# A new opening for a convolution and two fused MLPs on one core: taps by way of TensorE, the first convolution split between VectorE and TensorE

## The reference

```
w   = softmax(weight, axis=-1)                       # weight [8 heads, 7 taps]
out[b,s,h,g] = sum_k w[h,k] * x_pad[b, s+k, h, g]    # causal convolution over s, 24 channels a head
h1  = out.reshape(8192,192) @ w_in ;  g1 = max(0.01*h1, h1) ;  y1 = g1 @ w_out
h2  = y1 @ w_in2
g2  = h2 where h2>=1, 0 where h2<=-1, else (h2+1)**2/4
result = g2 @ w_out2                                 # d_model 192, d_ff 2048, x [2,4096,192] float32
```

## Time and profile before

| | |
|---|---|
| median of 3 runs | 1127.24 us (1127.17 to 1127.33) |
| the profiled execution | 1128.94 us, of which the span from first to last instruction is 1127.2 us |
| TensorE busy | 99% of the span, 9754 matmuls |
| VectorE busy | 80% |
| ScalarE busy | 71% |
| mean granted TensorE clock | 0.997 |

### The profile page before, as it was taken

The page is one execution under the profiler, slowest core; times in us unless marked ns, Lnnn a source line. Parts: engine busy times, 40 slices in busy tenths (PEclk is TensorE's granted clock), DMA queues, the critical chain, the costliest instruction groups (busy, mean ns, idle before and its releaser), DMA issues.

```text
span 1127.2 us, 25736 instructions
## 1 busy us (share of the span) xinstructions
PE 1117.2 (99%) x9754; PEld 923.7 (82%) x9754; DVE 898.4 (80%) x1511; ACT 798.7 (71%) x1472; POOL 45.8 (4%) x76
## 2 busy tenths in 40 slices
PE   8999999999999999999999999999999999999998
PEld 7888888888888888888888888888888888888886
DVE  6888887888777887788877888787788877888666
ACT  5878667586775867758577685866758677686785
POOL 4452000000000000000000000000000000000000
PEclk8999999999999999999999999999999999999999
DMA  6430010101001010010100101001010100100001
GB/s 132 109 77 6 14 17 1 30 2 25 6 1 30 1 29 1 1 30 1 29 1 8 23 1 29 1 13 18 1 29 1 24 7 1 29 1 15 1 1 29
DMA packets 114568, 21.98 MB, mean 19 GB/s; under 512 B 106256, under 2 KB 114448, under 8 KB 114448
## 3 DMA queue, kind: packets, MB, share of 16 engines
q1 hardware_dynamic: 111600, 19.61, 9.7%
q10 hardware_dynamic: 2848, 0.75, 0.4%
HBM read 14.05 MB, written 6.29 MB: 18 GB/s over the span
## 4 chain that ended last, share of the span: by engine, by line
PE 96%; DVE 2%; ACT 1%; issue 0%; DMA 0%; DVEq 0%
PE hidden L435 15%; PE hidden L429 10%; PE hidden L431 10%; PE hidden L433 10%; PE acc_main L499 10%; PE acc_main L501 10%; PE acc_edge L493 10%; PE acc_edge L490 10%; PE acc_main L503 10%; DVE g L958 0%; DVE acc_main L905 0%; ACT pre L681 0%; DMA y_main<-in_weight_dram 0%; ACT g_hi L700 0%; PE hidden L451 0%
## 5 line engine op out<-in xcount | busy, mean ns | idle before, releaser
L700 ACT CAST g_hi<-g 128x512 fp32r<-128x512 f32 x510 | 299.4, 618 | 267.6 <-PE acc_main L531 199.6
L969 DVE TENSOR_TENSOR g_lo<-g,g_hi 128x512 fp32r<-128x512 f32 x510 | 333.4, 687 | 94.3 <-ACT g_hi L700 89.7
L963 DVE SCALAR_TENSOR_TENSOR g<-hidden,pre 128x512 f32<-128x512 f32 x256 | 176.6, 690 | 101.6 <-ACT pre L688 98.7
L435 PE MATMUL hidden<-op_edge,w_edge 64*128 64x512 f32 x768 | 257.0, 388 | 0.0
L429 PE MATMUL hidden<-op_hi,w_main 64*128 64x512 f32 x512 | 198.6, 388 | 1.7 <-ACT op_hi L727 1.5
L447 PE MATMUL hidden<-op_hi,w_main 64*128 64x512 f32 x512 | 198.7, 388 | 0.0
L431 PE MATMUL hidden<-op_lo,w_main 64*128 64x512 f32 x512 | 198.7, 388 | 0.0
L451 PE MATMUL hidden<-op_hi,w_main 64*128 64x512 f32 x512 | 198.4, 388 | 0.0
L449 PE MATMUL hidden<-op_lo,w_main 64*128 64x512 f32 x512 | 198.4, 387 | 0.0
L433 PE MATMUL hidden<-op_hi,w_main 64*128 64x512 f32 x512 | 198.4, 387 | 0.0
L456 PE MATMUL hidden<-op_edge,w_edge 64*128 64x512 f32 x512 | 198.1, 387 | 0.0
(11 more groups left out here) (128 smaller groups left out, 2776.2 us busy)
## 6 DMA issues: line engine op xcount, KB each, us to landing
x_in<-in_x_dram SPq DMA_DIRECT2D x67, 64.0 KB, 2.2
out_dram<-y_main SPq DMA_DIRECT2D x62, 64.0 KB, 1.8
stage<-in_moe_w_out_dram SPq DMA_DIRECT2D x15, 192.0 KB, 2.7
x_in_edge<-in_x_dram SPq DMA_DIRECT2D x66, 32.0 KB, 2.0
out_dram<-y_edge SPq DMA_DIRECT2D x32, 64.0 KB, 1.8
stage<-in_moe_w_in_dram SPq DMA_DIRECT2D x15, 128.0 KB, 2.3
stage<-in_moe_w_in_dram SPq DMA_DIRECT2D x30, 64.0 KB, 2.4
stage<-in_moe_w_out_dram ACTq DMA_DIRECT2D x1, 192.0 KB, 4.2
```

The costliest lines, as they stand in the source:

```text
L435: done = nc.tensor.matmul(h[:], w_edge[l][top, i - 3, cols], op_edge[l][b][top, :], start=False, stop=False)
L700: nc.scalar.copy(hi_of(n, c)[:], g[c % SLOTS][:]).then_inc(g_hi_ready, 1)
L969: nc.vector.tensor_tensor(lo_of(n, c)[:], g[c % SLOTS][:], hi_of(n, c)[:].bitcast(F32), ALU.subtract).then_inc(g_lo_ready, 1)
```

## The change

The taps load brings 8x7 numbers to 8 partitions. GpSimd makes two 0/1 masks (`head_of`, 8 x 128); TensorE multiplies them with the raw taps, so that each of 128 partitions holds the logits of its own main and its own edge head. The softmax is then over 2x7 numbers a partition. The table of the exponential is called for by an early activation on a zero.

ScalarE scales `same` by the main taps (`main_diag`), and TensorE makes the last 128 columns of tile 0's main convolution; VectorE makes the first 384, and rounds these itself. GpSimd scales `same` by the edge taps. The warming matmuls are 3 ahead of the logits and 7 behind them. Piece 0 of the weights is loaded on SyncE's queue but for one part; half of tile 1's main x on ScalarE's. Chunk 0's edge passes (i = 3, 4) go ahead of its main passes. Of tile 1 one tap is made early and six in job 0; the parts of its operand are waited for pass by pass.

```
-WARM = 16
+WARM = 3
+WARM_ON = 7
+SPLIT = 3 * T // 4
-EARLY_TAPS = 2
-JOB_0_MAIN_TAPS = {0: 2, 1: 3, 2: 4, 3: 5, 4: 6}
-JOB_0_EDGE_TAPS = {6: (0,), 8: (1,), 9: (2, 3), 10: (4,), 11: (5, 6)}
+JOB_0_MAIN_TAPS = {0: 1, 1: 2, 2: 3, 3: 4, 4: 5, 5: 6}
+JOB_0_EDGE_TAPS = {8: (0, 1), 9: (2, 3), 10: (4,), 11: (5, 6)}
...
@@ sync
-                sp.dma_start(s[:, 0:PW], w[0:P]).then_inc(loaded, 16)
+                if piece:
+                    sp.dma_start(s[:, 0:PW], w[0:P]).then_inc(loaded, 16)
...
             load_x_edge(EVEN, 0, parts=range(2))
+            load_weights(0)
             load_weights(1)
-            load_x_main(ODD, 0)
+            load_x_main(ODD, 0, parts=P // Q - 2)
             load_weights(2)
@@ gpsimd
-            nc.gpsimd.memset(own[:], 1.0).then_inc(own_step, 1)
...
+            nc.gpsimd.memset(head_of, 1.0).then_inc(head_step, 1)
+            main = head_of[:, 0, :]
+            edge = head_of[:, 1, :].rearrange("h (r c) -> h r c", r=2)
+            pool.wait_ge(head_step, 1)
+            nc.gpsimd.affine_select(out=main, in_=main, compare_op=ALU.is_ge, fill=0.0, base=0,
+                                    pattern=[[1, P]], channel_multiplier=-GROUP)
...
+            pool.wait_ge(same_step, 3)
+            pool.wait_ge(taps_ready, 1)
+            for i in range(TAPS):
+                nc.gpsimd.tensor_scalar(edge_diag[i], same, taps[:, 1, i:i + 1], None, ALU.mult
+                                        ).then_inc(edge_diag_ready, 1)
+            low_w_in(0)
+            low_w_in(1)
+            low_w_out(0)
+            low_w_in(2)
+            low_w_out(1)
+            low_w_out(2)
@@ tensor: top_first
             if is_number(n, 0) and c == 0:
+                begin, last = i == 3, 1
+                if i == 3:
+                    pe.wait_ge(edge_hi_ready, 2)
+                    pe.wait_ge(weights_hi, 2)
+                if i == 4:
+                    pe.wait_ge(weights_ready, 1)
                 if i == 0:
                     pe.wait_ge(main_rounded, 1)
-                    pe.wait_ge(weights_hi, 1)
+                    pe.wait_ge(first_rounded, 1)
...
+            if is_number(n, 1) and c == 0:
+                if i == 0:
+                    pe.wait_ge(main_rounded, 2)
+                if i == 1:
+                    pe.wait_ge(main_low_ready, 1)
                 if i == 3:
-                    pe.wait_ge(edge_hi_ready, 2)
+                    pe.wait_ge(edge_hi_ready, 5)
@@ tensor: bottom_first, i == 3
-                if is_number(n, 0) and c == 0:
-                    pe.wait_ge(op1_ready, 1)
+                if is_number(n, 0, 1) and c == 0:
+                    pe.wait_ge(op1_ready, n + 1)
@@ tensor: opening
-            for i in (0, 2, 1, 3, 4):
+            for i in (3, 4, 0, 2, 1):
@@ tensor: ahead of the edge convolution
+            pe.wait_ge(head_of_ready, 1)
+            pe.wait_ge(taps_loaded, 16)
+            for a in (0, 1):
+                nc.tensor.matmul(logits[:, a, :], head_of[:, a, :], taps_raw, start=True, stop=True
+                                 ).then_inc(logits_ready, 1)
+            keep_warm(WARM_ON)
+            pe.wait_ge(x_turned, 1)
+            for i in range(TAPS):
+                pe.wait_ge(main_diag_ready, i + 1)
+                last = nc.tensor.matmul(last_main, main_diag[i], x_main[0][:, SPLIT + i:T + i],
+                                        start=i == 0, stop=i == TAPS - 1)
+            last.then_inc(last_convolved, 1)
@@ scalar
-            act.dma_start(taps_raw[:], weight.partition_broadcast(P)).then_inc(taps_loaded, 16)
+            act.dma_start(taps_raw, weight).then_inc(taps_loaded, 16)
...
+            act.wait_ge(warm_ready, 1)
+            nc.scalar.activation(exp_of_zero, g[0][:, 0:1], ACT.Exp)
...
             for i in range(TAPS):
-                nc.scalar.activation(edge_diag[i], same, ACT.Copy, scale=taps[:, 1, i:i + 1]).then_inc(edge_diag_ready, 1)
-                if i == 4:
-                    move_half((0, EVEN, 0))
+                nc.scalar.activation(main_diag[i], same, ACT.Copy, scale=taps[:, 0, i:i + 1]).then_inc(main_diag_ready, 1)
+            move_half((0, EVEN, 0))
+            for q in (2, 3):
+                act.dma_start(x_in[ODD][Q * q:Q * (q + 1), :].rearrange("r (g c) -> r g c", c=Q),
+                              x_rows[:, S // Q:S // Q + GROUPS, Q * q:Q * (q + 1)]).then_inc(x_loaded[ODD], 16)
             round_weights(0)
-            round_weights(1)
-            first_hi()
+            round_w_in(1)
             edge_hi((0, EVEN, 0))
+            last_hi()
             edge_low((0, EVEN, 0))
             edge_top((0, EVEN, 0))
+            round_w_out(1)
             round_weights(2)
@@ vector
-            dve.wait_ge(taps_loaded, 16)
-            nc.vector.reduce_max(taps_max[:], taps_raw[:], AX_X).then_inc(taps_step, 1)
+            dve.wait_ge(logits_ready, 2)
+            nc.vector.reduce_max(taps_max, logits, AX_X).then_inc(taps_step, 1)
...
-            nc.vector.tensor_tensor(own_inv[:], own[:, 0:2, :], taps_inv[:].unsqueeze(1).to_broadcast([P, 2, H]),
-                                    ALU.mult).then_inc(taps_step, 1)
...
-            nc.vector.reduce_sum(taps[:], own_taps[:].rearrange("p s h i -> p s i h"), AX_X).then_inc(taps_ready, 1)
+            nc.vector.tensor_tensor(taps[:], taps_exp, taps_inv.unsqueeze(2).to_broadcast([P, 2, TAPS]),
+                                    ALU.mult).then_inc(taps_ready, 1)
...
+                nc.vector.tensor_copy(op_hi[LEAKY][EVEN][:, first_part], first_main).then_inc(main_rounded, 1)
...
             for i in range(1, TAPS):
                 first_tap(i)
+            first_hi()
             first_lo()
-            edge_lo_first(first)
-            edge_lo_second(first)
+            last_lo()
+            edge_lo(first)
             turn_x_main(second)
-            for i in range(EARLY_TAPS):
-                main_tap(second, i)
+            main_tap(second, 0)
```

More of the change, by code:

```diff
@@ L126, in in_y_main @@
                 return part
[L127 to L140, removed]
+            return part.rearrange("p (a b) -> p a b", b=shape[1])
+        head_of = in_y_main(2, P)[0:H]
+        taps_raw = in_y_main(TAPS)[0:H]
+        taps_max = in_y_main(2)
+        taps_sub = in_y_main(2, TAPS)
+        taps_exp = in_y_main(2, TAPS)
+        taps_sum = in_y_main(2)
+        taps_den = in_y_main(2)
+        taps_inv = in_y_main(2)
+        exp_of_zero = in_y_main(1)
         hidden = [psum(f"hidden{i}") for i in range(SLOTS)]
@@ L253, in bass_conv_mlp_mlp @@
         edge_diag = [g[1 + i // 4][:, (i % 4) * P:(i % 4 + 1) * P] for i in range(TAPS)]
-        first_main = acc_main[0][:]
+        main_diag = [pre[i // 4][:, (i % 4) * P:(i % 4 + 1) * P] for i in range(TAPS)]
+        first_part, last_part = slice(0, SPLIT), slice(SPLIT, T)
+        first_main = acc_main[0][:, first_part]
+        last_main = hidden[3][:, 0:T - SPLIT]
+        logits = hidden[1][:, 0:2 * TAPS].rearrange("p (a b) -> p a b", b=TAPS)
         first_edge = acc_edge[0][:, 0:HALF]
@@ L379, in _, with low_w_in @@
                                     pattern=[[-1, P]], channel_multiplier=1).then_inc(same_step, 1)
-            made_after = {piece: CHUNKS * n + c + 1 for n in (0, 1) for c, piece in PIECE_AT[n].items()}
[L382 to L385, removed]
+            pool.wait_ge(same_step, 3)
[3 more added lines that the diff above has]
+                                        ).then_inc(edge_diag_ready, 1)
+            def low_w_in(piece):
+                s, main, edge, _, _ = piece_parts(piece)
                 pool.wait_ge(weights_hi, 3 * piece + 1)
@@ L390, in _, with low_w_out @@
                                         ALU.subtract).then_inc(weights_ready, 1)
+            def low_w_out(piece):
+                _, _, _, rows, wo = piece_parts(piece)
                 pool.wait_ge(weights_hi, 3 * piece + 3)
@@ L424, in top_first @@
                 if i == 0:
-                    if c == 0 and not is_number(n, 0):
+                    if c == 0 and not is_number(n, 0, 1):
                         pe.wait_ge((op1_ready, op2_ready)[l], t + 1)
@@ L758, in edge_top, with round_w_in @@
                 nc.scalar.copy(op_top[LEAKY][b][EDGE:P, 0:HALF], e).then_inc(op1_top_ready, 1)
-            def round_weights(piece):
-                s, main, edge, rows, wo = piece_parts(piece)
+            def round_w_in(piece):
+                s, main, edge, _, _ = piece_parts(piece)
                 act.wait_ge(stage_loaded[piece % AHEAD], 64 * (piece // AHEAD + 1))
```

97 lines of the change are left out of this document (52 added, 45 removed).

## The result

The changed kernel took 1125.52 us (median of 20 runs, 1124.89 to 1126.32), the kernel before beside it 1127.39 us (20 runs, 1127.01 to 1130.5). The ratio is 0.9978, with an interval of 0.9971 to 0.9984: faster by 0.22%. Applied to the 1127.24 us of the table that is 1124.8 us; forecast were 1123.1 us, with 1121.9 to 1125.4. This ratio follows the means, and seven long runs of the kernel before (1128.4 to 1130.5) raise its mean. By the medians the ratio is 0.9983 and the gain 1.9 us, against 4.1 us forecast; 1125.52 us itself lies 0.1 us above the range. The profiled execution took 1125.48 us, with a span of 1123.8 us, so the time around the span is 1.7 us as before.

A forecast was written before the change was run, and what follows sets the result against it. It took the kernel as an opening, then one unbroken TensorE stream. Earlier chunk 1 1.54, first chunks 2.26 and job 1 0.36, less 0.1 stalls, give 4.1 us off 1127.2: 1123.1 us, range 1121.9 to 1125.4.

The forecast's parts named there:

- the last of the sum: Final step: took 1123.1 us, the profiled span less the gain of 4.1, as forecast for the median.
- nothing, or up to 0.3 of stalls: Job 0: two edge taps at chunk 8 put 0.45 us into VectorE's chain; cost taken as 0.1 us.
- Taps: Opening: the small load, logits and shorter softmax have the taps ready at 5.0 us instead of 6.37.
- Transpose: VectorE's opening: x lands at 6.0 us, so the transpose starts at about 6.0 instead of 6.29.
- the prediction's own sign: Opening: if the transpose starts under 5.5 us, x was not late by nature.
- 128 columns: TensorE's opening: seven matmuls for tile 0's last 128 main columns take 1.95 us, some of it slow, to 8.7.
- chunk 1: Start of the stream: chunk 1 begins at 14.05 us, 1.54 us earlier than 15.59.
- fourth second-product pass: First chunk pair: VectorE lets this pass go at 20.1 us instead of 23.90; gain then 3.8 us.
- Waits pass by pass: Job 1's start: the new waits ask for parts that are long there; gain 0.36 us.
- Rival 1: Clock falls again after TensorE's pause from 12.05 to 12.9 us: gain 2.9 or 1.8, 1124.3 or 1125.4 us; chance 28%.
- Rival 2: Feeding late: x or weight pieces land later, or GpSimd's scalings cost over 0.9 us; 1124.5 us; chance 12%.
- Rival 4: Slower: short warming leaves the clock at half; 1129.6 us if it rises at 21.1 as before; chance 4%.

The follow-up runs named there:

- experiment 1: The kernel before, unchanged, run again on the first chip: 1127.64 us (10 runs, 1126.27 to 1128.15); profiled span 1126.0 us.
- experiment 2: The kernel before with five warming matmuls on zeros between the edge convolution and the first pass (the bridged kernel): 1126.34 us, ratio 0.9991.
- experiment 6: The changed kernel with tile 1's edge taps spread 1, 2, 1, 3 over chunks 8 to 11, one at chunk 8 instead of two: 1125.24 us.
- experiment 10: The kernel before with five matmuls on zeros in TensorE's pause at 12 us and job 1's operand waited for pass by pass, third chip: 1126.86 us.
- experiment 3: The changed kernel with 4 instead of 7 warming matmuls behind the logits, first chip: 1125.31 us (11 runs, 1124.82 to 1126.71).
- experiment 5: The changed kernel, unchanged, run again on the second chip: 1125.56 us (11 runs, 1124.79 to 1126.02), ratio 0.9982.
- experiment 7: The changed kernel with job 1's first pass again waiting for the whole operand of tile 1, second chip: 1126.93 us (11 runs).
- experiment 11: The changed kernel with chunk 0's main passes ahead of its edge passes, as in the old order, third chip: 1126.72 us (11 runs, two groups).

## Why the prediction was right, and where it was not

**The mechanism held.** An opening, then one unbroken stream; the start of the stream sets the end. Job 1's first pass and the end of the span lie 1079.6 to 1079.8 us apart in all 14 profiles (47.40 and 1127.2; 46.22 and 1126.0; 44.04 and 1123.8; 43.62 and 1123.4, and so on). That the result lies in the range is in part luck all the same. The measured gain is 1.9 us by the medians and 2.4 by the ratio, about half of the 4.1 forecast. The ratio of the medians would make 1125.4 of the 1127.24, the very end of the range.

**The step that was wrong is the last of the sum**: "the median 1127.24 happens to be near the span, so the forecast for the median is 1123.1". 1123.1 was a span. The profiled execution took 1.7 us more than its span, the changed one too, so the same sum gives an execution of 1124.8; measured were 1125.5. The median lay 1.7 us under the profiled execution not by chance but because most executions of the kernel before lose less than that one did: 0, 3.4 or 6.8 us at half clock, and 1126.3, 1127.7 or 1128.9 us by that on the first chip (experiments 1 and 2; the 0 is seen in the bridged kernel, whose times are those of the first group). A gain that is in part clock given back can't be taken from the median whole: it is there only as far as the median run had lost it. Of the 2.4 us between 1123.1 and 1125.5 this step is 1.7. On which chip the 1128.94 and the 1127.24 were taken is not on record: 1128.94 is not among the 20 runs beside the result, and a run of this time and span is among the 33 of the first chip. So a difference between chips may be in the 1.7 us too.

**The other 0.7 is a term of the sum**: "nothing, or up to 0.3 of stalls", taken as 0.1. It was 0.67 (3.70 to 3.03), and the edge taps of chunk 8 are its cause: with one tap there instead of two, 0.55 of it came back (experiment 6). The other tenth or so is spread over the terms before it. The forecast put 0.45 us of new work against a lead "of 0.6 or more"; two rests of 0.65 us lie behind the taps in the same queue, and TensorE's waits for them (0.49 and 0.31) show that the lead was smaller than that; the prediction had no row for it at this place.

**Term by term.** Taps: forecast 5.0, measured about 5.2. Two of their terms were off and cancelled in part: the logits took 1.02 us, not 0.4, and the steps behind them 1.44 (3.74 to 5.18), not 1.7. A matmul of 7 columns is far from free at half clock: the four records of the two cost 0.25 us each, as much as those of 128 columns (3.36 us for 14), and four weight loads of 0.23 us stand beside them. Transpose: 6.0 against 5.15, which by the prediction's own sign says that x was not late by nature. In the kernel before, too, it was the taps that let the transpose go: in experiment 10 they came 0.7 us later and the transpose followed them by the same 0.27 us as in the earlier trace rows. The time won here was not used, for TensorE was still warming until 6.99 (experiment 3): VectorE was no longer the one waited for. 128 columns: 1.95 against 2.23 (1.86 in experiment 5, 2.65 in 6). Edge convolution ended: 12.05 against 12.04. First pass: 12.9 against 12.88; chunk 1: 14.05 against 14.14; fourth second-product pass: 20.1 against 20.20. Rounding on VectorE: 0.5 against 0.56; GpSimd's scalings 0.58, between the bounds of 0.29 and 0.72. Waits pass by pass: 0.36 against 0.33 in the profiles (3.36 - 3.03); but in the changed kernel their absence costs 0.84 in the profiles and 1.4 on the medians (experiment 7), which the prediction did not see, since it priced them in the old stream.

**The rivals.** Rival 1 (the clock falls again) did not happen in the changed kernel; it did in about half of the runs of experiment 11, whose profile has a pause of 1.19 us, and probably in one run of experiment 3, so it was a near miss. By the Trainium skill (TensorE: Matmul & The Clock Gate, Part 1) the gate follows recent activity; experiments 2 and 11, where nothing but the pause and the order of the first passes was changed, agree. Rival 2 (feeding) did not happen. Rival 4 (a late rise) appeared in 4 of 11 runs with 64 columns, at a cost of 2.5 us.

**What the change is worth, by parts.** On the first two chips, where the kernel before has a median of 1127.7: the clock held, 1.35 us (experiment 2); the waits, 0.4 (experiment 10; the earlier trace rows); what remains, some 0.4 after what chunk 8 takes away, is the earlier start. On the third chip the earlier start is worth more, since the broadcast is slow there. The last two figures set chips beside each other and are no more than inferences; the changed kernel itself was not timed on the first and the third chip. In the series that gave the result, 13 of the 20 runs of the kernel before lie at 1127.0 to 1127.7 and 7 at 1128.4 to 1130.5, which looks more like the third chip; how its 1.9 us divide is therefore open.

## What to carry to other kernels

Before a sum is made against a profile, take a second and a third execution of the kernel: if its time comes in groups, subtract from each group what the change gives that group, and compare span with span. A stream of matmuls behind a pause of about 1.2 us may run its first microseconds at half clock in some executions only. Five matmuls on zeros in the pause settled it in experiment 2, and a first operand ready 0.5 us sooner did in the changed kernel; look for an earlier pause as well (experiment 10). And where the stream is brought forward, price anew each wait and each piece of work behind it, for the slack that hid them was measured against the old start.

## What the runs showed of the hardware

- The same program had times in three groups, on the first two chips 1.2 to 1.4 us apart, and the granted clock of 14 to 21 us tells their profiles apart. By the times, a pause of 1.46 us (kernel before) was followed by a fall in about two thirds of the runs on the first two chips, one of 1.19 us in 5 or 6 of 11. A pause of 0.85 us (nine profiles) or one of 0.36 us (one) was followed by none.
- The stretches at half clock lasted 3.4 us in three profiles (15.0 to 18.4, 14.9 to 18.3, 9.4 to 12.8) and 6.8 us in the fourth (14.3 to 21.1). Such a stretch cost less than half of its length: 1.4 us for 3.4, 2.6 for 6.8.
- The rise is as uncertain: the same seven matmuls with 128 columns at about 7 us took from 1.86 to 2.65 us. At half clock the columns of a small float32 matmul hardly count: a record took 0.25 us with 7 columns, 0.22 with 64 and 0.24 with 128, each with a weight load of about 0.22 beside it. In the records of these stretches the granted clock reads 1.00, and the slow matmuls show only by their durations.
- A broadcast of 28 KB to 128 partitions landed in 3.2 to 3.3 us in the profiles of two chips and in 3.9 us in the one of a third; the load of 56 numbers to 8 partitions, issued at 0.8 us, had landed by 2.7 us on all three.
- GpSimd multiplies 128x128 float32 numbers by a number for each partition in 0.58 us (seven in 4.08).
